# The last wait, the early routing and one weight piece moved in an xLSTM and mixture-of-experts kernel

## The chip, the core and the metric

The kernel runs on one core of a Trainium2 chip. A core has five engines with queues of their own: TensorE (PE), VectorE (DVE), ScalarE (ACT), GpSimd (POOL) and SyncE (SP, which only issues transfers here). The metric is the device time of one execution in microseconds (us), lower is better.

## What is computed

The input of the second stage is the output of the first.

```python
# stage 1, for B=2 batches, H=8 heads, S=768 steps, D=40
m_new = max(f + m, i);  C = exp(f+m-m_new)*C + exp(i-m_new)*outer(v, k);  n = the same with k
x = sigmoid(o) * (C @ q) / max(abs(n @ q), 1)          # x: [B, S, 320]
# stage 2, E=8 experts of width F=1024
logits = x @ w_gate;  local = sigmoid(x @ w_local)
e = argmax(logits) if s == 0 or local < 0.5 else the e of the step before
out[b, s] = softmax(logits)[e] * (relu(x @ w1[e]) @ w2[e])
```

## The kernel before

**Stage 1** goes through the sequence in six chunks (0 to 5) of 128 steps for all 16 pairs of batch and head. In a chunk TensorE makes exponents (`exponents(j)`, four quarters of four heads), ScalarE takes their exponentials, TensorE makes `scores`, VectorE multiplies both (`weigh(j)`), and TensorE makes the output of each quarter (`own_part(j)`, which reads the chunk's values) and what comes from the state (`old_part`). VectorE takes the outputs out of psO and adds both (`combine`, line 1459), keeps the state (`decay_state`, `add_state`) and makes x of the chunk before at the start of the next (`make_x`).

**Weights.** Every expert's weights come as five float32 pieces of 512 or 640 KB. ScalarE makes the float16 high half of a piece (`split_high`), VectorE the low half (`split_low`, line 1778), and only then is its staging slot free. `split_low` counts `weight_lows_ready` (s_wl) up by one. Pieces 0 to 19 are experts 0 to 3. The chunks do some of the low halves between their own steps: pieces 0 to 3 in chunk 1, 4 to 7 in chunk 2, 8 to 11 in chunk 3, 12 and 13 in chunk 4, 14 in chunk 5.

**Transfers.** SyncE issues its transfers in the order of the program, and a wait holds all that stand behind it. The loop of chunk c issues queries and keys of chunk c+1, the rows of x of chunk c-2, then a weight piece, then the values, keys and output gates of chunk c+1 (`in_kvo`, 968 KB), then the other pieces of `LOADS[c]`. A piece's load waits until the last user of its slot has its low half. So piece 8, the last load of chunk 1's loop, waits for the low half of piece 3 (s_wl 4); in chunk 2's loop piece 9 waits for that of piece 4, and the last, 12, for that of piece 7; piece 16, the last of chunk 3's loop, waits for that of piece 11 (s_wl 12), and piece 17, with the values of chunk 5 right behind it, for that of piece 12 (s_wl 13). Piece 18 waits for that of piece 15.

**GpSimd** scales the keys and splits the rows of exponents of the next chunk; `SPLIT_AT` is the count of low halves after which it starts the splitting. Later it gathers tiles of tokens from the x rows in HBM and writes tiles of the output, both by indirect transfers.

**Routing** of tokens to experts is made by VectorE with small products on TensorE. For chunks 0 to 2 it is done early, in chunks 4 and 5: `early_choice`, `early_fill` (needs the keys turned by TensorE), `early_codes` (needs TensorE's product of the codes), `early_slots` (needs that of the ranks), `early_sources`. The last writes `srcid`, with which GpSimd gathers the first tile. Then the same is done for all tokens (`route_choice`, `route_fill`, `route_codes`, `route_ranks`, `route_slots`).

**Stage 2** takes tiles of 128 tokens of one expert: `first_up` or `up` (up projection), relu, for the last tiles a `turn` (eight transposes) of the hidden row, then `down`, 24 products with float16 high and low halves of hidden and weights. The output tile is scaled and written by GpSimd.

```python
            turn(n3 + 2)                        # TensorE, the last tile
            idle(psM[:], GAP["last"])           # five products that nobody reads
            down(n3 + 2, e, halves=True)
            # GpSimd, after its last write
            pool.wait_ge(s_out, 16 * n3 + 48)
            pool.sem_inc(s_done, 1)
```

## Time and profile before

| | us |
|---|---|
| median of 3 runs (lowest, highest) | 232.96 (232.5, 234.62) |
| the profiled execution | 232.61 |
| its span, first to last instruction | 230.8 |
| TensorE matmul busy | 216.1 (94%) |
| VectorE busy | 168.1 (73%) |
| ScalarE busy | 122.8 (53%) |
| GpSimd busy | 68.2 (30%) |

The span is 1.8 us shorter than the time of the same execution. Stage 1 takes the first 97 us of the span, the routing of all tokens stands between 105 and 124 us under the first tiles, and the tiles run until 224 us. The mean granted clock of TensorE over the span is 0.996 of full speed.

### The profile page before, as it was taken

The numbers are of one execution on the slowest core, as the hardware profiler recorded it, in microseconds if no ns is written. First come the engines' busy times: TensorE is split into PE (matmuls) and PEld (weight loads), VectorE is DVE, ScalarE is ACT, GpSimd is POOL, SyncE is SP. The second block draws the span as 40 slices with busy tenths as digits, with TensorE's granted clock in tenths as the row PEclk, the third lists the DMA queues.
The fourth block names the chain that finished last, engine by engine and source line by source line (L and its number), as shares of the span: only waits on it lengthen the run. The fifth ranks groups of instructions, "written<-read, shape, count | busy, mean of one in ns | idle before, by whom it ended". The sixth has DMA issues, their size and how long they took to land.

```text
span 230.8 us, 5934 instructions
## 1 busy us (share of the span) xinstructions
PE 216.1 (94%) x2276; PEld 174.4 (76%) x2277; DVE 168.1 (73%) x348; ACT 122.8 (53%) x212; POOL 68.2 (30%) x77
## 2 busy tenths in 40 slices
PE   4998999999999899999999999999999999999970
PEld 1566878788888778899778698998889967666640
DVE  5599999999998989888898869998687630322130
ACT  2231769786968765455346727776666233334110
POOL 1043080260442430530013815431352332321021
PEclk9999999999999999999999999999999999999998
DMA  5999839999999720038940896896253011010000
GB/s 145 296 259 380 326 78 366 257 356 367 280 408 247 242 99 3 17 95 258 417 164 21 235 388 186 310 318 244 62 147 145 0 41 43 29 39 3 9 28 25
DMA packets 12840, 42.30 MB, mean 183 GB/s; under 512 B 2181, under 2 KB 4288, under 8 KB 12812
## 3 DMA queue, kind: packets, MB, share of 16 engines
q1 hardware_dynamic: 10812, 37.40, 48.4%
q0 software_dynamic: 1824, 4.35, 5.8%
q8 instruction: 19, 0.31, 0.6%
q10 hardware_dynamic: 176, 0.17, 0.3%
q14 instruction: 9, 0.07, 0.1%
HBM read 38.37 MB, written 4.98 MB: 188 GB/s over the span
## 4 chain that ended last, share of the span: by engine, by line
PE 73%; DVE 15%; DMA 4%; issue 3%; ACT 1%; POOL 0%; DVEq 0%; POOLq 0%
PE psU L1230 20%; PE psO L1049 7%; PE psO L1198 7%; PE psS L1198 6%; PE psS L1212 6%; PE psS L1019 4%; PE psU L1029 3%; PE psU L1101 2%; PE psU L899 2%; DVE W L1778 2%; PE psM L960 2%; PE psA L1000 2%; DMA stage<-in_w 2%; PE psA L1003 2%; PE psA L1005 2%
## 5 line engine op out<-in xcount | busy, mean ns | idle before, releaser
L1230 PE MATMUL psU<-W,hidT 128*128 128x320 f16 (+1 forms) x360 | 51.5, 299 | 0.1
L1230 PEld LDWEIGHTS psU<-W,hidT 128*128 128x128 f16 x360 | 35.0, 98 | 13.4 <-issue 0.5
L606 POOL DMA_INDIRECT out<-rows,srcid x11 | 15.1, 1375 | 56.3 <-ACT rows L828 56.0
L1049 PEld LDWEIGHTS psO<-W,hidT 128*128 128x128 f32 x192 | 24.1, 191 | 3.3 <-DVE hidT L1439 2.3
L1049 PE MATMUL psO<-W,hidT 128*128 128x82 f32 x192 | 25.6, 274 | 1.0 <-DVE W L1454 0.7
L1198 PE MATMUL psO<-xT,W 128*128 128x128 f16 x384 | 22.9, 219 | 0.0
L1198 PEld LDWEIGHTS psO<-xT,W 128*128 128x128 f16 x384 | 21.9, 98 | 0.4
L728 ACT ACTIVATE hid<-psA 128x512 f32<-128x512 f32 x24 | 14.2, 591 | 14.6 <-PE psA L1005 14.3
L1439 DVE TENSOR_TENSOR hidT<-psS,hid 128x512 f32<-128x512 f32 x24 | 16.4, 685 | 3.8 <-PE psS L1019 3.7
L558 POOL TENSOR_TENSOR W<-W 128x640 f32<-128x640 f32 x5 | 6.3, 1262 | 43.3 <-DVE W L1740 30.9
L1716 DVE TENSOR_TENSOR xT<-psM,xT 128x384 f16<-128x384 f32 x13 | 7.2, 557 | 14.7 <-ACT xT L720 14.6
L1198 PE MATMUL psS<-xT,W 128*128 128x128 f16 x256 | 15.1, 219 | 0.0
L1198 PEld LDWEIGHTS psS<-xT,W 128*128 128x128 f16 x256 | 14.6, 98 | 0.2
L1212 PE MATMUL psS<-W,xT 128*128 x64 | 14.5, 379 | 0.0
L1778 DVE SCALAR_TENSOR_TENSOR W<-W 128x1280 f16<-128x1280 f32 (+1 forms) x10 | 14.4, 1436 | 0.1
L1019 PE MATMUL psS<-W 40*128 40x128 f32 x192 | 13.9, 285 | 0.4 <-DVE hidT L1439 0.4
L1019 PEld LDWEIGHTS psS<-W 40*128 40x128 f32 x192 | 11.6, 187 | 3.2 <-issue 2.4
L828 ACT ACTIVATE rows<-psU,ptile 128x320 f32<-128x320 f32 x14 | 7.4, 527 | 10.9 <-PE psU L1230 8.1
L1778 DVE SCALAR_TENSOR_TENSOR W<-stage,W 128x1024 f16<-128x1024 f32 (+1 forms) x10 | 12.6, 1267 | 0.0
L662 ACT ACTIVATE W<-stage 128x1024 f16<-128x1024 f32 (+1 forms) x10 | 10.9, 1095 | 2.4 <-DMA stage<-in_w 2.4
L720 ACT CAST xT<-psM 128x384 f16<-128x384 f32 x13 | 6.2, 477 | 10.9 <-PE psM L1135 10.7
L662 ACT ACTIVATE W<-W 128x1280 f16<-128x1280 f32 (+1 forms) x10 | 11.8, 1180 | 0.1
(259 smaller groups left out, 436.3 us busy)
## 6 DMA issues: line engine op xcount, KB each, us to landing
W<-in_w SPq DMA_DIRECT2D x10, 512.0 KB, 5.5
W<-in_w SPq DMA_DIRECT2D x8, 640.0 KB, 6.5
W<-in_qk SPq DMA_DIRECT2D x12, 416.0 KB
W<-in_kvo SPq DMA_DIRECT2D x5, 968.0 KB, 7.6
stage<-in_w SPq DMA_DIRECT2D x9, 512.0 KB, 7.0
stage<-in_w SPq DMA_DIRECT2D x7, 640.0 KB, 7.3
rows<-in_w SPq DMA_DIRECT2D x5, 512.0 KB, 6.1
x_rows<-rows SPq DMA_DIRECT2D x12, 192.0 KB, 7.8
```

Of the source, the lines that this page charges most:

```text
L606: pool.indirect_dma_start(out[:, :], bass.IndirectOffsetOnAxis(ap=rows_of, axis=0), ybuf, None, bounds_check=TOK - 1, oob_is_err=False).th ...
L662: nc.scalar.activation(high(e, i), staged(n), ACT.Copy, scale=WSC).then_inc(s_wh, 1)
L728: nc.scalar.activation(wexp[j % 2], psA[:, j % 2], ACT.Exp).then_inc(s_exp, 1)
L828: nc.scalar.activation(ybuf, psU[:, 0:DM], ACT.Copy, scale=ptile[:, bass.ds(t, 1)]).then_inc(s_yk, 1)
L1019: last = mm(psS[:, a, h * P:(h + 1) * P], kstack[u][r, g], qstack[u][r, g], start=True, stop=True)
L1049: last = mm(psO[:, j % 2, h * V:(h + wide) * V], prob[j % 2][:, h], values, start=True, stop=True)
L1198: last = mm(at, W1[:, home(t), part, f * P:(f + 1) * P], x[:, k * P:(k + 1) * P], start=(n == 0), stop=(n == len(terms(t)) - 1))
L1212: last = mm(psS[:, half], x[:, k * P:(k + 1) * P], w, start=(n == 0), stop=(n == len(terms(t)) - 1))
L1230: return mm(psU[:, 0:DM], h[:, k * P:(k + 1) * P], w, start=(h is hi and part == 0 and k == 0), stop=(h is lo and k == FC - 1))
L1439: vv.tensor_tensor(prob[j % 2].rearrange("p h t -> p (h t)"), psS[:, j % 2], wexp[j % 2], ALU.mult).then_inc(s_p, 1)
L1716: vv.tensor_tensor(l, ps[:, 0:KC * P], h, ALU.subtract).then_inc(s_xte, 1)
L1778: vv.scalar_tensor_tensor(out=low(e, i), in0=staged(n)[p], scalar=WSC, in1=high(e, i)[p], op0=ALU.mult, op1=ALU.subtract).then_inc(s_wl, 1)
```

## The change

Five edits.

1. At the end VectorE, not GpSimd, waits for the last output writes.
2. The low half of piece 3 moves from chunk 1 to chunk 2, and with it one piece on every later boundary: chunk 1 does 0 to 2, chunk 2 does 3 to 6, chunk 3 does 7 to 10, chunk 4 does 11 and 12, chunk 5 does 13 and 14. `SPLIT_AT` goes down by one with it.
3. In chunk 4 TensorE makes the early codes after the state update and not ahead of `own_part(2)`, and the early ranks after the first scores of chunk 5 and not ahead of `own_part(3)`; each has a semaphore of its own. VectorE does `early_fill` after `combine(0)`, and `early_norms` at the end of chunk 5.
4. In the routing of all tokens VectorE does `route_fill` ahead of the first hidden low half and `route_codes` ahead of the early gates, and TensorE makes the slots one group of eight products later.
5. The last turn signals its first half, ScalarE starts on that, and the five idle products are gone.

```diff
-SPLIT_AT = (0, 0, A_CHUNK + 2, 2 * A_CHUNK + 2, 3 * A_CHUNK + 1)
+SPLIT_AT = (0, 0, A_CHUNK + 1, 2 * A_CHUNK + 1, 3 * A_CHUNK)
...
             for t in range(3):
                 write(n3 + t)
-            pool.wait_ge(s_out, 16 * n3 + 48)
-            pool.sem_inc(s_done, 1)
...
             def last_hidden_high(t):
-                act.wait_ge(s_ht, t + 1)
                 act.wait_ge(s_yh, t)
                 act.wait_ge(s_hk, t)
                 for half in range(2):
+                    act.wait_ge(s_ht, t + 1 + half)
...
-                mm(at_last1, r1["onesr"], r1["lastd"], start=True, stop=True)
+                mm(at_last1, r1["onesr"], r1["lastd"], start=True, stop=True).then_inc(s_cd1, 1)
...
                 pe.wait_ge(s_rv1, R1_OHB)
+                pe.wait_ge(s_oc, NQ * (NC - 1))
...
-                    if c == NC - 2 and j == 2:
-                        early_codes()
-                    if c == NC - 2 and j == 3:
-                        early_ranks()
...
                 scores(0)
+                if c == NC - 1:
+                    early_ranks()
...
                     last.then_inc(s_u, 1)
+                if c == NC - 2:
+                    early_codes()
...
-            def turn(t):
+            def turn(t, halves=False):
...
+                    if halves and k == FC // 2 - 1:
+                        last.then_inc(s_ht, 1)
...
-            first_up(3, {4: slots})
+            first_up(3, {5: slots})
...
-            turn(n3 + 2)
+            turn(n3 + 2, halves=True)
             e = expert(n3 + 2)
-            idle(psM[:], GAP["last"])
             down(n3 + 2, e, halves=True)
...
-                piece = A_CHUNK * (c - 1)
+                piece = A_CHUNK * (c - 1) - 1
...
                     combine(1)
-                    split_low(3)
                     return
...
                     weigh(2)
-                    early_fill()
                     combine(0)
                     scale_old(1)
                     keep_logits(2 * (c - 1))
+                    early_fill()
+                    weigh(3)
                     split_low(piece + 1)
-                    weigh(3)
                     early_codes()
...
-                    early_norms()
+                    split_low(piece - 2)
                     early_sources()
...
-                    split_low(piece - 2)
+                    split_low(piece - 1)
                     combine(1)
+                    early_norms()
...
+            route_fill()
             first_hidden_low(0)
-            route_fill()
             tile_low(2)
+            route_codes()
             early_gates()
-            route_codes()
             early_slot_gates()
             make_scale(NC - 1)
+            keep_gates(ptile[:, 0:LAST_E], at_gates1, s_gp1)
+            first_hidden_low(1)
             split_low(17)
-            first_hidden_low(1)
-            keep_gates(ptile[:, 0:LAST_E], at_gates1, s_gp1)
...
             result(n3 + 2)
+            dve.wait_ge(s_out, 16 * n3 + 48)
+            dve.sem_inc(s_done, 1)
```

VectorE from the end of chunk 1 to its first low half of chunk 2 (W is the memory of weights and attention, hidT holds the weighted scores, lg the logits). Before:

```order
L1459 TENSOR_TENSOR W<-psO,W 128x328 [waits old_part_scaled,outputs_ready]
L1778 SCALAR_TENSOR_TENSOR W<-W 128x4x320 [waits weight_highs_ready]
L1722 SCALAR_TENSOR_TENSOR W<-W 128x16 [waits outputs_taken]
L1725 TENSOR_SCALAR W<-W 128x16 [waits norm_bound_ready]
L1727 RECIPROCAL W<-W 128x16 [waits norm_bound_ready]
L1733 TENSOR_TENSOR W<-W 128x16x40 [waits norm_ready]
L1439 TENSOR_TENSOR hidT<-psS,hid 128x512 [waits outputs_ready,exp_done,scores_ready]
L1740 SCALAR_TENSOR_TENSOR W<-th,W 128x640 [waits x_transposed,x_rows_kept,output_gate_ready,normed_ready]
L1429 COPY lg<-psM 128x9 [waits logits_product_ready]
L1439 TENSOR_TENSOR hidT<-psS,hid 128x512 [waits outputs_ready,exp_done,scores_ready]
L1447 TENSOR_TENSOR W<-psU,W 128x328 [waits outputs_taken,old_part_ready]
L1778 SCALAR_TENSOR_TENSOR W<-W 128x4x320 [waits weight_highs_ready]
```

In the changed kernel:

```order
L1460 TENSOR_TENSOR W<-psO,W 128x328 [waits old_part_scaled,outputs_ready]
L1723 SCALAR_TENSOR_TENSOR W<-W 128x16 [waits outputs_taken]
L1726 TENSOR_SCALAR W<-W 128x16 [waits norm_bound_ready]
L1728 RECIPROCAL W<-W 128x16 [waits norm_bound_ready]
L1734 TENSOR_TENSOR W<-W 128x16x40 [waits norm_ready]
L1440 TENSOR_TENSOR hidT<-psS,hid 128x512 [waits outputs_ready,exp_done,scores_ready]
L1741 SCALAR_TENSOR_TENSOR W<-th,W 128x640 [waits x_transposed,x_rows_kept,output_gate_ready,normed_ready]
L1430 COPY lg<-psM 128x9 [waits logits_product_ready]
L1440 TENSOR_TENSOR hidT<-psS,hid 128x512 [waits outputs_ready,exp_done,scores_ready]
L1448 TENSOR_TENSOR W<-psU,W 128x328 [waits outputs_taken,old_part_ready]
L1779 SCALAR_TENSOR_TENSOR W<-W 128x4x320 [waits weight_highs_ready]
```

The instruction of line 1778 behind the last `combine` (the low half of piece 3) is gone there, and the one at the end of the second list, after `weigh(1)` and `scale_old(0)`, is now that of piece 3; SyncE's queue has no row moved.

TensorE in chunk 4 from the logits on (psO<-cfs,rows and psO<-W,rows are the codes, psU<-W 64x41 the state update). Before:

```order
L960 MATMUL psM<-W,xT 128x81 [waits x_transposed_kept,exp_done]
L960 MATMUL psM<-W,xT 128x81 x2
L973 MATMUL psO<-cfs,rows 128x6 [waits early_route_step,outputs_taken,weighted_scores_ready]
L974 MATMUL psO<-W,rows 128x6
L1049 MATMUL psO<-W,hidT 128x82 x4
L948 MATMUL psM<-cfs,W 128x128 [waits logits_kept,logits_product_ready,consts_loaded,decay_ready]
L948 MATMUL psM<-cfs,W 128x128
L948 MATMUL psM<-cfs,W 64x128
L1101 MATMUL psU<-W 64x41 [waits old_part_scaled,scaled_keys_ready]
L1101 MATMUL psU<-W 64x41 x15
L1000 MATMUL psA<-cbf,W 128x512 [waits exp_done,split_rows_ready]
```

In the changed kernel:

```order
L959 MATMUL psM<-W,xT 128x81 [waits x_transposed_kept,exp_done]
L959 MATMUL psM<-W,xT 128x81 x2
L1045 MATMUL psO<-W,hidT 128x82 [waits outputs_taken,weighted_scores_ready]
L1045 MATMUL psO<-W,hidT 128x82 x3
L947 MATMUL psM<-cfs,W 128x128 [waits logits_kept,logits_product_ready,consts_loaded,decay_ready]
L947 MATMUL psM<-cfs,W 128x128
L947 MATMUL psM<-cfs,W 64x128
L1099 MATMUL psU<-W 64x41 [waits old_part_scaled,scaled_keys_ready]
L1099 MATMUL psU<-W 64x41 x15
L972 MATMUL psO<-cfs,rows 128x6 [waits early_route_step]
L973 MATMUL psO<-W,rows 128x6
L1000 MATMUL psA<-cbf,W 128x512 [waits exp_done,split_rows_ready]
```

The two codes products now stand behind the state update, and `own_part(2)` follows the logits directly.

VectorE in chunk 4 from the low half ahead of `weigh(2)` to the first step of the codes. Before:

```order
L1778 SCALAR_TENSOR_TENSOR W<-W 64x1024 [waits weight_highs_ready]
L1439 TENSOR_TENSOR hidT<-psS,hid 128x512 [waits outputs_ready,exp_done,scores_ready]
L1611 TENSOR_SCALAR rows<-psO 6x128 [waits outputs_ready]
L1612 SCALAR_TENSOR_TENSOR rows<-rows,psO 6x128 [waits early_route_step]
L1613 TENSOR_SCALAR W<-cfs,rows 6x6 [waits early_route_step]
L1459 TENSOR_TENSOR W<-psO,W 128x328 [waits old_part_scaled,outputs_ready,x_ready,early_route_step]
L1447 TENSOR_TENSOR W<-psU,W 128x328 [waits outputs_taken,old_part_ready]
L1429 COPY lg<-psM 128x9 [waits logits_product_ready]
L1778 SCALAR_TENSOR_TENSOR W<-W 128x4x320 [waits weight_highs_ready]
L1439 TENSOR_TENSOR hidT<-psS,hid 128x512 [waits outputs_ready,exp_done,scores_ready]
L1618 TENSOR_SCALAR W<-psO 128x6 [waits outputs_ready]
```

In the changed kernel:

```order
L1779 SCALAR_TENSOR_TENSOR W<-stage,W 128x1024 [waits weight_highs_ready]
L1440 TENSOR_TENSOR hidT<-psS,hid 128x512 [waits outputs_ready,exp_done,scores_ready]
L1460 TENSOR_TENSOR W<-psO,W 128x328 [waits old_part_scaled,x_ready,outputs_ready]
L1448 TENSOR_TENSOR W<-psU,W 128x328 [waits outputs_taken,old_part_ready]
L1430 COPY lg<-psM 128x9 [waits logits_product_ready]
L1612 TENSOR_SCALAR rows<-psO 6x128 [waits outputs_ready]
L1613 SCALAR_TENSOR_TENSOR rows<-rows,psO 6x128 [waits early_route_step]
L1614 TENSOR_SCALAR W<-cfs,rows 6x6 [waits early_route_step]
L1440 TENSOR_TENSOR hidT<-psS,hid 128x512 [waits exp_done,outputs_ready,scores_ready,early_route_step]
L1779 SCALAR_TENSOR_TENSOR W<-W 64x1024 [waits weight_highs_ready]
L1619 TENSOR_SCALAR W<-psO 128x6 [waits early_codes_turned]
```

`combine(0)` (W<-psO,W) now stands three steps earlier, and the second low half, whose end is s_wl 13, stands behind `early_fill` and `weigh(3)`.

## Rows read from the trace of the kernel before

**Rows 1.** The page: the chain of waits by engine, share of the span.

```profile
PE 73%; DVE 15%; DMA 4%; issue 3%; ACT 1%; POOL 0%; DVEq 0%; POOLq 0%
```

**Rows 2.** Timeline, VectorE, chunk 2: start us, us, instruction.

```profile
41.82 0.68 DVE L1439 TENSOR_TENSOR hidT<-psS,hid 128x512 f32<-128x512 f32 x1
...
44.23 1.78 DVE L1778 SCALAR_TENSOR_TENSOR W<-W 128x1280 f16<-128x1280 f32 x1
```

**Rows 3.** Timeline, TensorE, the start of chunks 2 and 3.

```profile
39.68 1.16 PE L1019 MATMUL psS<-W 40*128 40x128 f32 x16
...
42.56 1.12 PE L1049 MATMUL psO<-W,hidT 128*128 128x82 f32 x8 [0.23 <-DVE hidT L1439]
...
57.05 1.09 PE L1049 MATMUL psO<-W,hidT 128*128 128x82 f32 x8
```

**Rows 4.** Timeline, SyncE's queue, chunks 1, 2 and 4.

```profile
40.48 0.33 SPq L473 DMA_DIRECT2D W<-in_w  x1
...
46.42 0.58 SPq L463 DMA_DIRECT2D W<-in_kvo  x1
...
76.81 0.33 SPq L473 DMA_DIRECT2D W<-in_w  x1
...
77.18 0.43 SPq L463 DMA_DIRECT2D W<-in_kvo  x1
```

**Rows 5.** DMA issues from 40.3 on (piece 8): KB, us to landing.

```profile
W<-in_w SPq DMA_DIRECT2D x1, 640.0 KB, 5.5
```

**Rows 6.** DMA issues at 103.7 (piece 18).

```profile
stage<-in_w SPq DMA_DIRECT2D x1, 640.0 KB, 4.6
```

**Rows 7.** DMA issues at 46.4 (values of chunk 3).

```profile
W<-in_kvo SPq DMA_DIRECT2D x1, 968.0 KB, 8.5
```

**Rows 8.** DMA issues at 77.1 (values of chunk 5).

```profile
W<-in_kvo SPq DMA_DIRECT2D x1, 968.0 KB, 5.9
```

**Rows 9.** Busy time from 41 to 54: us, PE busy, clock, DMA share, GB/s.

```profile
41.00:54.00 13.00, 12.77 (x135) 1.00 0.95 322
```

**Rows 10.** Timeline, TensorE, chunk 4 and the start of chunk 5.

```profile
79.24 0.19 PE L973 MATMUL psO<-cfs,rows 6*128 6x6 f32 x1 [0.88 <-DVE W L1459]
...
87.58 0.38 PE L903 MATMUL psA<-cbf 128*128 128x512 bf16 x1
```

**Rows 11.** Timeline, VectorE, chunk 4.

```profile
77.42 0.27 DVE L1611 TENSOR_SCALAR rows<-psO 6x128 f32<-6x128 f32 x1
...
78.64 0.50 DVE L1459 TENSOR_TENSOR W<-psO,W 128x328 f32<-128x328 f32 x1
...
79.73 1.48 DVE L1778 SCALAR_TENSOR_TENSOR W<-W 128x1280 f16<-128x1280 f32 x1
```

**Rows 12.** Timeline, VectorE, the low half of the first tile.

```profile
98.65 0.56 DVE L1716 TENSOR_TENSOR rows<-psA,rows 128x384 f16<-128x384 f32 x1 [0.70 <-ACT rows L720]
```

**Rows 13.** Timeline, TensorE: first gathered tile, keys, slots.

```profile
97.55 0.55 PE L1135 MATMUL psA<-cfs,xt 128*128 128x128 f32 x3 [0.21 <-DMA xt<-x_rows,srcid]
...
108.17 0.27 PE L1152 MATMUL psA<-cfs,W 128*12 128x128 f32 x1
...
123.77 0.46 PE L1168 MATMUL psA<-W 128*128 128x16 bf16 x12 [0.52 <-DVE W L1898]
```

**Rows 14.** Timeline, VectorE, the first low half of a hidden tile.

```profile
107.96 1.22 DVE L1800 SCALAR_TENSOR_TENSOR hidT<-psS,hidT 128x1024 f16<-128x1024 f32 x1
```

**Rows 15.** Timeline, the last tile: ScalarE and GpSimd.

```profile
219.29 1.07 ACT L820 CAST hidT<-psO 128x512 f16<-128x512 f32 x2 [3.11 <-PE psO L1220]
...
225.25 0.98 POOL L606 DMA_INDIRECT out<-rows,outid  x1 [2.38 <-DVE rows L1818]
```

**Rows 16.** Chain of waits, the last tile: start us, us, what.

```profile
218.38 0.87 PE psO L1220 x8
...
219.26 1.08 PE psM L908 x5
```

**Rows 17.** The instructions after the last line of the program, GpSimd.

```profile
L98 POOLq DRAIN  x1: 2770/2770/2770, 227.8 to 227.8; - x1
```

More of the change, by code:

```diff
@@ L67 @@
 LOADS = {1: (5, 6, 7, 8), 2: (9, 10, 11, 12), 3: (13, 14, 15, 16), 4: (17, 18)}
-GAP = dict(tile=1, last=5)
+GAP = dict(tile=1)
 BIG = 2.0 ** 30
@@ L72 @@
 G_L0, G_B0, G_L1, G_A1, G_B1, G_L, G_A, G_B, G_EG = 5, 12, 16, 18, 19, 23, 25, 26, 27
-R1_KEY, R1_SUB, R1_KEPT, R1_OHB, R1_HOT, R1_SRC, R1_END = 8, 9, 12, 17, 28, 34, 44
+R1_KEY, R1_SUB, R1_KEPT, R1_OHB, R1_HOT, R1_SRC, R1_END = 8, 9, 12, 17, 28, 30, 44
 R_KEY, R_SUB, R_CODE, R_OHB, R_HOT, R_SRC, R_REST, ROUTE_STEPS = 10, 11, 14, 19, 46, 48, 67, 73
@@ L303, in build @@
         s_yh = sem("high_products_done")
+        s_cd1, s_rk1 = sem("early_codes_turned"), sem("early_ranks_ready")
         s_cb, s_tab = sem("bf16_consts_loaded"), sem("router_weights_loaded")
@@ L973, in early_codes @@
                 nc.tensor.transpose(at_code1, r1["coder"], const("ident")[0:N1, 0:N1])
-                mm(at_last1, r1["onesr"], r1["lastd"], start=True, stop=True)
+                mm(at_last1, r1["onesr"], r1["lastd"], start=True, stop=True).then_inc(s_cd1, 1)
             def early_ranks():
                 pe.wait_ge(s_rv1, R1_OHB)
+                pe.wait_ge(s_oc, NQ * (NC - 1))
                 mm(at_later1, trib, r1["ohb"][:, 0:LAST_E * N1], start=True, stop=True)
-                mm(at_total1, sel_ones, r1["ohb"][:, 0:LAST_E * N1], start=True, stop=True)
+                mm(at_total1, sel_ones, r1["ohb"][:, 0:LAST_E * N1], start=True, stop=True).then_inc(s_rk1, 1)
             def early_slots():
@@ L1660, in early_codes @@
             def early_codes():
-                dve.wait_ge(s_o, NQ * (NC - 2) + 3)
+                dve.wait_ge(s_cd1, 1)
                 carry(early, r1, N1, at_code1, at_last1)
@@ L1666, in early_slots @@
             def early_slots():
-                dve.wait_ge(s_o, NQ * (NC - 1))
+                dve.wait_ge(s_rk1, 1)
                 hot_of = r1["ohb"][:, 0:LAST_E * N1]
```

## The prediction

> **What bounds the kernel now.** I read the chain of waits first, then the timelines of TensorE and VectorE side by side over stage 1, then SyncE's queue, then the last tile. The chain is TensorE for 73% of the span, VectorE 15%, transfers 4% [rows 1]: work that TensorE does itself can't be touched by this change, so what it can win is the idle time between. The reader is to see four such places. At the start of chunk 2 TensorE waits 0.23 for the first weighted scores [rows 3]. In chunk 4 it waits 0.88 for `combine(0)` [rows 10]. At the slots it waits 0.52 [rows 13]. In the last tile five products that nobody reads take 1.08 [rows 16]. After the program GpSimd drains for 2.77 [rows 17]. No transfer stops TensorE in stage 1 except the first gather, 0.21 [rows 13], but SyncE's queue was hardly ever empty: from 41 to 54 the DMA engines were 95% busy at 322 GB/s [rows 9].
>
> **The change part by part.** A minus is time saved; positions are those of the profiled execution.
>
> Chunk 1. The low half of piece 3 stood on VectorE ahead of `make_x` and `weigh(0)` of chunk 2, which started at 41.82 [rows 2]; a low half of that form takes 1.48 [rows 11]. Without it `weigh(0)` starts when the scores are there: they start at 39.68 and take 1.16 [rows 3], so at 40.9. TensorE then has its filling products, and `own_part(0)` starts at 42.15, not 42.56: the 0.23 of idle and the rest that the model of the matmul ends hides. Term: **-0.4**.
>
> SyncE's queue, the price of the move. The low half also frees a slot. SyncE issued piece 8 at 40.48 [rows 4], when that of piece 3 ended. Now this low half stands where that of piece 4 stood, at 44.23 [rows 2], less the 0.9 that VectorE is ahead: it runs from 43.3 and ends, with 1.5 to 1.8 for it, at 45.0. Queries and keys of chunk 3, the rows, piece 9 and the values of chunk 3 are queued behind piece 8, and all move by 4.5 at first. Before, the values were issued at 46.42 and landed 8.5 later, at 54.9 [rows 4, 7], 14.4 after the issue of piece 8; of these 0.9 were an older backlog (piece 8 took 5.5 to land, a like piece in an empty queue 4.6 [rows 5, 6]). So upper bound: 45.0 + 13.5 = 58.5. Lower bound: these transfers are 3.55 MB (640, 832, 384, 640 and 968 KB), at 322 GB/s [rows 9] 11.0, and 1 for the start: 57.0. I take 58.0, nearer to the upper, which is the same list in the same order. `own_part(0)` of chunk 3 needs the values, at 57.05 before [rows 3], at 56.65 now. Term: **+1.3** (0.4 to 1.9), a new wait of TensorE on a transfer; it stands at +0.9 then.
>
> Chunk 4 has the same queue (piece 12 now waits for a low half of chunk 3), but its values come at 71 to 72.5 by the same sum from 59.5, and TensorE, 0.9 late, asks for them at about 72.4: nothing.
>
> Chunk 4, codes and ranks. `early_fill` took from 77.42 to 78.64 and `combine(0)` came after it [rows 11]; TensorE waited 0.88 for it until 79.24 and made the codes before `own_part(2)` [rows 10]. Now `combine(0)` is first, `own_part(2)` can start when the logits end, 1.3 earlier, and the two groups of small products come back later at 0.2: **-1.1**. VectorE gives back half of this, since it does the same list, but one low half is 1.22 and not 1.48; it is not late at the next chunk.
>
> Chunk 5, the same queue again. Piece 17 went at 76.81 and the values at 77.18, landing 5.9 later, at 83.1 [rows 4, 8]; TensorE asked for them at 87.58 [rows 10], so 4.5 were to spare. Now s_wl 13 is the second low half of chunk 4. From 77.42: `combine(0)`, `scale_old`, logits 1.1 (78.64 to 79.73 [rows 11]), `early_fill` 1.2, `weigh(3)` 0.6, low half 1.25, end 81.6. Values go at 82.05, land at the earliest at 87.95 (5.9 [rows 8]), plus the 0.9 by which all is late: 88.9. Upper bound: piece 16 now goes at 76.8, where piece 17 went, and with queries, keys, rows, piece 17 and values it is 3.29 MB, by the same rate as in chunk 3 (13.5 for 3.55) 12.5: 89.3, and 90.2 with the 0.9. I take 89.5, the middle. TensorE is then 1.9 later than at 87.58 before; without the wait it would be at 0.9 - 1.1 = 0.2 earlier. Term: **+2.1** (1.5 to 2.8). The spare time is spent because the wait moved past a whole block of `early_fill`, `weigh` and a low half.
>
> The Trainium skill bears on this: "DMA: Bandwidth & Descriptors", section on the anatomy of one DMA, gives for a GpSimd transfer about 2.0 us fixed plus bytes over 436 GB/s. By that estimate the 968 KB land 4.3 after issue, or 5.5 with the 512 KB ahead of them, and the wait of chunk 5 nearly vanishes; the row shows 5.9.
>
> End of chunk 5. `early_sources` gets a low half of 1.48 before it and loses `early_norms` (0.85) and a wait of 0.2; the gather that follows ended a wait of 0.21 [rows 13]: +0.15. `early_norms` now stands between `combine(1)` and the first tile's low half, where VectorE waited 0.70 for ScalarE [rows 12]: 0.85 is 0.2 too much. Together **+0.35** (0 to 0.6).
>
> All tokens' routing. Eight products later are 0.45 against the wait of 0.52 [rows 13]. But VectorE now waits for the keys before the first hidden low half: it started that at 107.96 [rows 14], the keys only ran at 108.17 for 0.27 [rows 13], so 0.5 is idle where before 0.2 was (for tile 2's high half). The slots come 0.3 later. Term: **-0.25** (-0.5 to 0).
>
> Last tile. Before, ScalarE began at 219.29 after the whole turn, two copies in 1.07 [rows 15], and the five products took 1.08 from 219.26 [rows 16]. The turn took 0.87 for eight transposes [rows 16]; now the first four are enough: ScalarE starts at 218.85, its half is there at 219.4, and `down` starts at 219.45, not 220.33. VectorE's half is needed 16 products later. Term: **-0.85**.
>
> The end. The last indirect transfer runs at 225.25 for 0.98 [rows 15], GpSimd sees it landed and only then drains, 2.77 from 227.8 [rows 17]. Now it can drain from 226.25 while the data are on the way, and VectorE sees them when GpSimd did. Not shown is a drain with a transfer in flight: if it waits for that, 0 is gained; if not, 1.55. GpSimd had nothing to run for 1.5 before its drain and it still took 2.77, so it isn't left-over work: I take **-1.55**.
>
> Sum: -0.4 + 1.3 - 1.1 + 2.1 + 0.35 - 0.25 - 0.85 - 1.55 = -0.4. The profiled execution's 232.61 gives 232.2; the median of the runs is 0.35 above it, so 232.5. About 1% is what a measurement of this kernel can tell from no change.
>
> **Rivals.**
> (a) The transfers are hidden. For it: 4.5 were to spare in chunk 5, and an emptied queue may be quicker than a full one. Against it: the 5.9 was already in a nearly empty queue. Then there are no +1.3 and little of +2.1, TensorE is 1.5 ahead at chunk 5, VectorE's path to the gather only 0.9: -0.9 - 0.25 - 0.85 - 1.55 = -3.5, 229.5. The page's rule above leads here.
> (b) Slower: the queue of SyncE costs its upper bounds. Chunk 3's values at 58.5 make TensorE 1.45 late, chunk 5's then come at 90.75, 3.2 late: 3.2 + 0.35 - 0.25 - 0.85 - 1.55 = +0.9, 233.9. It decides from a landing of chunk 5's values after 89.9. For it: queries and keys come in the middle of the list each time.
> (c) GpSimd's drain waits for the transfer: 1.55 not gained, 234.0.
> (d) The new order doesn't remove the wait of chunk 4, since VectorE is the bound there: +1 on the forecast, but most of that would only shorten the wait on chunk 5's values. It hardly changes the sum.
>
> **How the numbers follow.** Forecast 0.53 (232.5, from 231 to 233.5 by the terms' bounds), (a) 0.18, (b) 0.14, (c) 0.15. The range from 229.7 to 234.2 leaves out about half of (a) and the worst of (b) and (c). Faster by over 1% (below 230.6) is (a) and a little of the forecast, 0.22; slower by over 1% (above 235.3) is (b) and (c) together, 0.1; the rest, 0.68, within 1%.
>
> **What the profile after would show.** SyncE's queue: piece 8 at 45, the values of chunk 5 at about 83. TensorE: waits for `in_kvo` at the first own part of chunk 3 (about 1.3) and chunk 5 (about 2), none for `combine(0)` in chunk 4, still one at the slots of some 0.5, and none of the five products. GpSimd's drain starting near the end of its last transfer. I am wrong above all if these two waits on the values aren't there, or if the drain ends where it did.

## The result: slower, 244.2 us

| | before | changed |
|---|---|---|
| median of 6 runs each (lowest, highest), us | 232.8 (232.5, 234.62) | 244.17 (240.16, 245.3) |
| ratio, 95% interval | | 1.0385 [1.03, 1.047] |
| the profiled execution | 232.61 | 244.6 |
| its span | 230.8 | 242.8 |
| mean granted clock of TensorE | 0.996 | 0.954 |

The ratio is made only from runs within 1.5% of the fastest of each kernel (240.16, 242.18 and 243.74 us of the changed one), so it lies below that of the two medians, and the profiled 244.6 us is one of the three left out. The forecast was 232.5 us, within 229.7 to 234.2: it was wrong by 11.7 us.

I read the profile after in the order of before. First the chain of waits by engine, for [rows 1]:

```profile
PE 70%; DVE 13%; DMA 11%; issue 3%; SPq 1%; POOLq 1%; ACT 0%; DVEq 0%; ACTq 0%
```

Transfers went from 4% of the chain to 11%. The chain in order of time names them, two loads of `in_kvo` (start us, us, what):

```profile
50.27 11.97 DMA W<-in_kvo
...
89.29 9.14 DMA W<-in_kvo
```

Next SyncE's queue, for [rows 4]. A group of issues of one line is one row: start of the first, us until the end of the last.

```profile
38.92 8.81 SPq L474 DMA_DIRECT2D W<-in_w  x2
47.82 0.36 SPq L455 DMA_DIRECT2D W<-in_qk  x1
...
50.27 0.47 SPq L464 DMA_DIRECT2D W<-in_kvo  x1
...
74.86 9.43 SPq L474 DMA_DIRECT2D stage<-in_w  x2
84.39 0.35 SPq L455 DMA_DIRECT2D W<-in_qk  x1
...
89.29 0.48 SPq L464 DMA_DIRECT2D W<-in_kvo  x1
```

Piece 8 is the second of the two issues from 38.92 on and ends at 47.73. Between them SyncE stands still for 8 us, with the queries and keys of chunk 3 and its values behind it. In chunk 3's loop the same happens to piece 16 (until 84.29), with chunk 5's queries, keys and values behind it. TensorE pays for both, for [rows 3, 10, 13]:

```profile
41.96 1.16 PE L1019 MATMUL psS<-W 40*128 40x128 f32 x16
...
62.29 2.00 PE L1045 MATMUL psO<-W,hidT 128*128 128x82 f32 x8 [3.43 <-DMA W<-in_kvo]
...
92.97 1.21 PE L1019 MATMUL psS<-W 40*128 40x128 f32 x16 [1.31 <-DMA W<-in_qk]
...
98.48 0.61 PE L902 MATMUL psA<-cbf 128*128 128x512 bf16 x1 [2.32 <-DMA W<-in_kvo]
...
111.32 0.55 PE L1135 MATMUL psA<-cfs,xt 128*128 128x128 f32 x3 [0.37 <-DMA xt<-x_rows,srcid]
...
138.10 0.46 PE L1168 MATMUL psA<-W 128*128 128x16 bf16 x12 [0.89 <-DVE W L1899]
...
233.54 3.52 PE L1232 MATMUL psU<-W,hidT 128*128 x24 [0.40 <-ACT hidT L819]
```

The three waits on transfers are 7.1 us. That is not all that was lost: the eight products of `own_part` that took 1.09 in [rows 3] take 2.00 here. The windows show why (us, then busy us of PE, PEld, DVE, ACT and POOL with counts, granted clock, DMA share, GB/s):

```profile
35.94:39.35 3.41, 3.41 (x42) 2.88 (x40) 3.28 (x7) 3.41 (x8) 0.00 (x0) 0.50 0.99 398
59.83:66.66 6.83, 4.37 (x21) 3.52 (x23) 3.65 (x7) 3.41 (x8) 4.02 (x5) 0.50 0.93 296
93.97:104.20 10.23, 7.91 (x46) 6.65 (x44) 4.45 (x16) 2.87 (x8) 0.41 (x1) 0.50 0.21 83
```

These are three stretches in which TensorE's granted clock is 0.50, that is 1.2 GHz and not 2.4. Two of them hold a wait on a transfer or follow one: the first fell after TensorE had waited some 1 us of its 3.43, the second 1 us after the wait on the keys. TensorE was busy for 15.7 us in the three; at full clock that would be about half, so by this estimate some 7.8 us are lost by the clock: 1.7 in the first stretch, which stands ahead of any wait on a transfer, and 6.1 in the other two. Before, the clock was at 0.50 only from 228.9 us on, after the last product.

The lag behind the profiled execution of before, at the same instruction in both, puts it together (my differences of the two traces' start times):

| place | before | changed | lag |
|---|---|---|---|
| transposes of x, chunk 1 | 34.77 | 35.54 | 0.77 |
| first scores of the next chunk | 39.68 | 41.96 | 2.28 |
| `own_part(0)`, chunk 3 | 57.05 | 62.29 | 5.24 |
| `own_part(0)`, chunk 4 | 71.53 | 78.81 | 7.28 |
| `own_part(3)`, chunk 4 | 82.92 | 89.06 | 6.14 |
| products ahead of `own_part(0)`, chunk 5 | 87.58 | 98.48 | 10.90 |
| first gathered tile | 97.55 | 111.32 | 13.77 |
| last `down` | 220.17 | 233.54 | 13.37 |
| end of the span | 230.8 | 242.8 | 12.0 |

The first 2.28 us are not the moved piece's doing: 0.77 stand there from the first products of the program on (5.86 us for 14 of them, 5.07 before), and 1.5 come with the first stretch at half clock; both belong to the section on the clock in chunk 1. The 1.1 that chunk 4 was to give is there (7.28 to 6.14), and 1.4 at the end too (13.37 to 12.0); from the first gathered tile to the last `down` it gains 0.4. Everything else loses.

The end, for [rows 15, 17] (GpSimd's last transfer, then the instructions after the program's last line):

```profile
238.71 0.98 POOL L607 DMA_INDIRECT out<-rows,outid  x1 [1.96 <-DVE rows L1819]
...
L98 POOLq DRAIN  x1: 4055/4055/4055, 238.5 to 238.5; - x1
L98 DVEq DRAIN  x1: 17/17/17, 241.3 to 241.3; - x1
```

From the start of the last transfer to the end of the span it is 4.1 us, where it was 5.55 (225.25 to 230.8).

### The profile page after: what moved, and what is told of

It is laid out like the page before. It is cut to its first block, busy times and chain, and to the rows that moved or that the text cites. A ratio compares the mean times of both kernels' runs of the same rounds, so it can differ in the third digit from the quotient of the medians.

```text
span 242.8 us, 5925 instructions
## 1 busy us (share of the span) xinstructions
PE 222.9 (92%) x2271; PEld 180.1 (74%) x2272; DVE 167.9 (69%) x348; ACT 123.5 (51%) x212; POOL 68.2 (28%) x77
## 3 DMA queue, kind: packets, MB, share of 16 engines
HBM read 38.37 MB, written 4.98 MB: 179 GB/s over the span
## 4 chain that ended last, share of the span: by engine, by line
PE 70%; DVE 13%; DMA 11%; issue 3%; SPq 1%; POOLq 1%; ACT 0%; DVEq 0%; ACTq 0%
PE psU L1232 19%; DMA W<-in_kvo 9%; PE psO L1198 8%; PE psS L1198 7%; PE psO L1045 6%; PE psS L1212 6%; PE psS L1019 4%; PE psU L898 2%; DVE W L1779 2%; PE psM L959 2%; PE psU L1029 2%; PE psA L1000 2%; PE psU L1099 2%; PE psA L1003 2%; PE psA L1005 2%
## 5 line engine op out<-in xcount | busy, mean ns | idle before, releaser
L1232 PEld LDWEIGHTS psU<-W,hidT 128*128 128x128 f16 x360 | 35.1, 98 | 13.5 <-issue 0.6
L1045 PE MATMUL psO<-W,hidT 128*128 128x82 f32 x192 | 27.2, 286 | 4.2 <-DMA W<-in_kvo 3.4
L1045 PEld LDWEIGHTS psO<-W,hidT 128*128 128x128 f32 x192 | 26.1, 204 | 6.4 <-DMA W<-in_kvo 3.6
L559 POOL TENSOR_TENSOR W<-W 128x640 f32<-128x640 f32 x5 | 7.4, 1481 | 53.8 <-DVE W L1741 31.2
L1019 PE MATMUL psS<-W 40*128 40x128 f32 x192 | 15.0, 299 | 1.8 <-DMA W<-in_qk 1.3
L1019 PEld LDWEIGHTS psS<-W 40*128 40x128 f32 x192 | 12.6, 201 | 5.0 <-issue 2.5
L591 POOL DMA_INDIRECT xt<-x_rows,srcid x6 | 7.9, 1323 | 14.7 <-DVE srcid L1694 12.4
L1029 PE MATMUL psU<-W 104*128 104x82 f32 x80 | 12.0, 297 | 0.0
```

What stands on the lines that cost most here:

```text
L591: pool.indirect_dma_start(xbufs[x_buffer(t)], None, xs[0:count], bass.IndirectOffsetOnAxis(ap=rows_of, axis=0), bounds_check=count - 1, oo ...
L1019: last = mm(psS[:, a, h * P:(h + 1) * P], kstack[u][r, g], qstack[u][r, g], start=True, stop=True)
L1029: last = mm(old.rearrange("p (a h) d -> p h a d", a=2)[:, i], qstack[u][0:PAIR, g], Cbd[0:PAIR, g], start=True, stop=True)
L1045: last = mm(psO[:, j % 2, h * V:(h + wide) * V], prob[j % 2][:, h], values, start=True, stop=True)
L1232: return mm(psU[:, 0:DM], h[:, k * P:(k + 1) * P], w, start=(h is hi and part == 0 and k == 0), stop=(h is lo and k == FC - 1))
```

## The experiments

The theories after the result: **the queue** (SyncE, held by the moved low halves, brings values and keys late, and TensorE's clock falls in the waits), against **VectorE's order** (codes, fill and norms in their new places make it late), against a clock that falls by itself. Each kernel was compared with runs of the kernel before on the same chip; its medians there were 234.85 us (beside the first four kernels), 234.74 (the next four) and 235.46 (the last three), higher than in the first comparison. What goes with that is told with the last runs.

### The weight piece put back, all else kept

```diff
-SPLIT_AT = (0, 0, A_CHUNK + 1, 2 * A_CHUNK + 1, 3 * A_CHUNK)
+SPLIT_AT = (0, 0, A_CHUNK + 2, 2 * A_CHUNK + 2, 3 * A_CHUNK + 1)
...
-                piece = A_CHUNK * (c - 1) - 1
+                piece = A_CHUNK * (c - 1)
...
                     combine(1)
+                    split_low(3)
...
-                    split_low(piece - 2)
                     early_sources()
...
-                    split_low(piece - 1)
+                    split_low(piece - 2)
```

> The changed kernel with the weight piece back where it was (low half of piece 3 in chunk 1, pieces of the later chunks as before); every other edit is kept. Theory 1, the queue: SyncE's list is held by the moved low halves, so chunk 3's and chunk 5's values (and chunk 5's keys) land late. Then TensorE's waits on transfers in chunks 3 and 5 (3.43, 1.31 and 2.32 us) and the stretches at half clock are gone, and what is left is the forecast's sum without -0.4, +1.3 and +2.1: +0.35 - 1.1 - 0.25 - 0.85 - 1.55 = -3.4, that is 229.4 us beside 232.8. Theory 2, VectorE: codes, ranks, fill and norms in the new order make VectorE late for TensorE in chunks 4 and 5, and the queue only follows it. Then some 240 us or more.

Measured: 232.24 us (229.34 to 232.34, 4 runs), ratio 0.9868 [0.9798, 0.9939]. TensorE's idle places from 33 to 110 us are two:

```profile
34.83 0.90 PE L947 MATMUL psM<-cfs,W 128*128 128x128 f32 x3 [0.63 <-DVE W L1424]
...
98.99 0.55 PE L1135 MATMUL psA<-cfs,xt 128*128 128x128 f32 x3 [0.28 <-DMA xt<-x_rows,srcid]
```

No wait on keys or values is left. The loss of the change is the moved piece; VectorE's order as the cause has fallen. The one run with a mean clock of 0.994 took 229.34, which is the forecast of 229.4; the other three had 0.982 to 0.983 and took 232.2 to 232.3. The profiled execution is one of the three: its clock was at 0.50 for 6.8 us in chunk 1. From `own_part(0)` of chunk 3 (59.61) to the end of its span (230.4) it is 170.8 us, before 173.8 (57.05 to 230.8): by positions the edits that are left gave 2.9 us and not 3.4, so that the 229.34 meets the forecast so closely is in part luck.

### The weight piece alone

The same lines the other way, on the kernel before.

> The kernel before with the weight piece moved and nothing else. Theory 1, the queue: the values of chunk 3 land some 12 us after their issue, late by 3 us or more, and chunk 5's also; the time is that of the changed kernel plus the 3.4 that the other edits give: some 247 us (244 to 249). Theory 2, VectorE's new order in chunks 4 and 5 is the cause: only chunk 3's wait is there, and the time is under 240 us.

Measured: 251.78 us (249.14 to 255.13, 4 runs), ratio 1.0622 [1.0543, 1.0701]. The waits, and then the window behind the first of them:

```profile
63.09 2.00 PE L1049 MATMUL psO<-W,hidT 128*128 128x82 f32 x8 [3.40 <-DMA W<-in_kvo]
...
100.97 1.16 PE L1019 MATMUL psS<-W 40*128 40x128 f32 x16 [0.76 <-DMA W<-in_qk]
...
106.38 0.61 PE L903 MATMUL psA<-cbf 128*128 128x512 bf16 x1 [3.20 <-DMA W<-in_kvo]
```

```profile
62.00:82.40 20.40, 19.31 (x117) 16.67 (x117) 8.22 (x14) 8.26 (x16) 4.88 (x6) 0.50 0.76 242
```

The waits are 7.4 us, against 7.1 in the changed kernel, so the moved piece makes them by itself. Two of the four runs took 249.1 and 249.3 us, at the upper end of my 244 to 249; the other two, the profiled one with 254.27 among them, lie above it. In that trace the clock was at 0.50 for 30.7 us in stage 1 and not for 20.5: 6.8 in chunk 1, 20.5 at the first wait (61.9 to 82.4), 3.4 at the end of the last one (106.3 to 109.7). The sum that I made from the changed kernel took the length of such a stretch for fixed, and it isn't.

### Values ahead of the pieces in SyncE's list

```diff
-LOADS = {1: (5, 6, 7, 8), 2: (9, 10, 11, 12), 3: (13, 14, 15, 16), 4: (17, 18)}
+LOADS = {1: (5, 6, 7), 2: (8, 9, 10, 11), 3: (12, 13, 14, 15), 4: (16, 17, 18)}
...
-                    load_piece(LOADS[c][0])
                     load_values(c + 1, (c + 1) % 2)
-                    for n in LOADS[c][1:]:
+                    for n in LOADS[c]:
```

> The changed kernel with SyncE's list turned round: each chunk's values ahead of its weight pieces, and the piece that had stood first in the list left for the next chunk (pieces 5-7, 8-11, 12-15, 16-18). VectorE's order is the changed one. Theory 1, the queue: the values are asked for early enough, TensorE doesn't wait for them in chunks 3 and 5, the clock stays at full, and the time is 229 to 231 us, if the last pieces are still there for the first tile. Theory 2, VectorE's order: the wait moves from the values to weighted scores or the state, and the time stays above 238 us.

Measured: 230.85 us (229.02 to 232.16, 4 runs), ratio 0.9834 [0.9758, 0.9909]. VectorE's order is the changed one, with the late low halves. SyncE now has the values of chunk 3 out at 42.2 and lets piece 8 wait behind them:

```profile
42.17 0.60 SPq L464 DMA_DIRECT2D W<-in_kvo  x1
47.60 2.19 SPq L474 DMA_DIRECT2D W<-in_w  x2
```

No wait on keys or values is in the trace, only one of 0.69 for the first gather (98.83). So it isn't the late low half that costs, but what stands behind it in the queue. From `own_part(0)` of chunk 5 to the first gather it is 10.25, and 9.82 in the kernel with the piece put back: the 0.4 are the low half that now stands ahead of `early_sources`.

### TensorE kept busy in the waits

```diff
+COVER = {3: 14, 5: 10}
...
+                    if c in COVER:
+                        fill(0, COVER[c])
                     pe.wait_ge(s_kvo[u], 16 * (k + 1))
```

> The changed kernel with products that nobody reads ahead of TensorE's wait for the values in chunk 3 (14 of them) and chunk 5 (10), so that TensorE is busy while it would wait. Theory A, the clock falls because TensorE stands still, and work after the wait pays for it: the two stretches at 0.50 (6.8 and 10.2 us) get shorter or vanish, and the time is 238 to 241 us. Theory B, the waits themselves are the whole price, or the clock falls for another reason: 244 us as before or more, with the stretches at 0.50 in their places.

Measured: 238.6 us (236.14 to 240.06, 4 runs), ratio 1.0134 [1.0057, 1.0212]. The profiled execution took 236.14; its clock was at 1.00 until the end:

```profile
59.83:66.66 6.83, 6.58 (x62) 5.81 (x62) 3.08 (x5) 5.06 (x10) 4.69 (x6) 1.00 0.89 246
93.97:104.20 10.23, 9.90 (x92) 8.54 (x89) 7.48 (x20) 4.37 (x12) 3.71 (x3) 1.00 0.07 18
```

TensorE in chunks 1 to 3 and at the start of chunk 5 (line 903 is the fill):

```profile
39.57 1.16 PE L1020 MATMUL psS<-W 40*128 40x128 f32 x16
...
42.05 1.01 PE L1046 MATMUL psO<-W,hidT 128*128 128x82 f32 x8
...
56.31 3.19 PE L903 MATMUL psA<-cbf 128*128 128x512 bf16 x14
60.08 1.12 PE L1046 MATMUL psO<-W,hidT 128*128 128x82 f32 x8 [0.58 <-DMA W<-in_kvo]
...
88.44 1.16 PE L1020 MATMUL psS<-W 40*128 40x128 f32 x16 [1.04 <-DMA W<-in_qk]
...
90.53 2.65 PE L903 MATMUL psA<-cbf 128*128 128x512 bf16 x11
93.01 1.01 PE L1046 MATMUL psO<-W,hidT 128*128 128x82 f32 x8
```

The same work runs 8.5 us shorter than the changed kernel's profiled execution (244.6) with 24 products more. Not all of that is the filling's: 0.9 us are the start of the program (14 products in 4.98 and 5.86 us), and some 1.7 the fall of the clock in chunk 1, which this execution didn't have. The medians are 5.6 us apart (238.6 and 244.17), near the 6.1 estimated for the two stretches after waits. The rest is the waits: 236.14 stands 6 to 7 us above the 229.0 and 229.8 of the profiled executions of the two mended kernels at the end of this section. So of the moved piece's loss about half is the clock and half the waits. This is also the trace that shows the waits without the clock in between: 3.7 us in chunk 3 (14 products of 0.22 and 0.58), 1.0 for the keys and some 2.2 for the values of chunk 5 (the values land at 92.7, and TensorE had nothing else to do from 90.5 on).

SyncE here issues piece 8 at 45.0 (a row of 38.04 with 7.30 for two issues) and the values at 47.97; they land 12.1 later, at 60.0.

### Four small edits, each alone on the kernel before

> The kernel before, with VectorE instead of GpSimd waiting for the last writes. Theory 1: GpSimd's drain runs beside its last transfer; from the issue of the last indirect transfer to the end of the program it takes 4.0 us, as in the changed kernel, where it was 5.55: -1.5 us. Theory 2: the drain gets longer by what it no longer waits beforehand, or VectorE's sight of the landing is later: 0. TensorE's last group ends at the same place in both.

Measured: 233.28 us (230.84 to 234.03, 12 runs), ratio 0.9922 [0.9872, 0.9971].

```profile
227.26 0.98 POOL L606 DMA_INDIRECT out<-rows,outid  x1 [2.36 <-DVE rows L1816]
...
L98 POOLq DRAIN  x1: 4081/4081/4081, 227.0 to 227.0; - x1
```

From 227.26 to the span's end of 231.3 it is 4.0, before 5.55: -1.5. The drain got longer, from 2.77 to 4.08, but not by what it no longer waits beforehand.

> The kernel before, with the last turn released in two halves and the five products that nobody reads taken out. Theory 1: TensorE's last products start 0.85 us earlier after the end of the first up products of that tile (ScalarE's copy of the first half no longer waits for the last four transposes): -0.8 us. Theory 2: without the five products TensorE stands still for some 0.5 us and the last products run at half clock for longer than before (3.9 us at the end of the kernel before): 0, or slower by up to 1.

Measured: 233.74 us (231.95 to 235.54, 12 runs), ratio 0.9968 [0.9919, 1.0018].

```profile
220.36 1.04 PE L1220 MATMUL psO<-cfs,hid 128*128 128x128 f32 x8
221.80 3.57 PE L1232 MATMUL psU<-W,hidT 128*128 x24 [0.40 <-ACT hidT L820]
```

From the turn's first transpose to `down` it is 1.44, before 1.95 (218.22 to 220.17): -0.5. ScalarE's copy began 0.72 after the turn's start and `down` 0.72 after that. The last products didn't run at half clock, and neither did they before: the 3.9 us of the expectation begin at 228.9, after the last product.

> The kernel before, with the early codes and ranks later on TensorE and the early fill behind the weighted sum on VectorE, without the moved weight piece. Theory 1: TensorE's wait of 0.88 us for the weighted sum in chunk 4 is gone and the first gather comes earlier by some 1 us: -0.8 to -1.1 us. Theory 2: VectorE's list is as long as it was and sets when the first gather's indices are ready, so that TensorE's wait moves to the gather (0.21 us before): -0.2 us at most.

Measured: 233.77 us (231.87 to 234.69, 12 runs), ratio 0.9962 [0.9919, 1.0004].

```profile
74.13 1.09 PE L1047 MATMUL psO<-W,hidT 128*128 128x82 f32 x8
...
89.22 1.01 PE L1047 MATMUL psO<-W,hidT 128*128 128x82 f32 x8
...
99.13 0.55 PE L1137 MATMUL psA<-cfs,xt 128*128 128x128 f32 x3 [0.37 <-DMA xt<-x_rows,srcid]
```

From `own_part(0)` of chunk 4 to that of chunk 5 it is 15.09, before 16.28 (71.53 to 87.81): -1.2, and 0.2 of it are given back at the gather (9.91 against 9.74).

> The kernel before with only the new order on VectorE after stage 1 (the keys' fill ahead of the first hidden low half, the codes ahead of the early gates) and the slots' products eight products later on TensorE. One look, for positions: from the first gathered tile's transposes (97.55 before) to the slots' products (123.77) it was 26.2 us, to the second tile's products (129.96) 32.4. Forecast's theory: the wait at the slots stays at some 0.5 and the way to 129.96 gets shorter by 0.25. Rival: VectorE waits for the keys for longer than it gains, the slots' wait grows to 0.9, as in the changed kernel's variants, and the way is not shorter (32.4 to 32.6).

Measured: 235.74 us, one run.

```profile
100.37 0.55 PE L1135 MATMUL psA<-cfs,xt 128*128 128x128 f32 x3 [0.31 <-DMA xt<-x_rows,srcid]
...
127.06 0.46 PE L1168 MATMUL psA<-W 128*128 128x16 bf16 x12 [0.88 <-DVE W L1898]
...
132.80 2.47 PE L1230 MATMUL psU<-W 128*128 128x320 f16 x17 [0.25 <-issue]
```

The way from the first gathered tile to the second one's products is 32.43, before 32.41. The slots' products stand eight products later and are still waited for, 0.88 instead of 0.52: the rival held. VectorE stood idle for 0.62 before the keys that it now takes first:

```profile
111.37 0.28 DVE L1611 TENSOR_SCALAR W<-psA 12x128 f32<-12x128 f32 x1 [0.62 <-PE psA L1152]
```

Of the three edits with twelve runs only the end's has an interval clear of 1; the sizes of the other two are from the traces.

### The clock in chunk 1

Runs of one kernel differed by 3 us. In eight of the ten profiles shown so far (all but that of the kernel before and that with the waits filled) the clock fell at 35 us of the span, at 34.6 to 36.5, for 3.4 or 6.8 us. A wait of 0.62 for VectorE stands there in every one, in the kernel before too. Three products, 0.65 us, were put in front of it, on each of three kernels:

```diff
+EARLY_COVER = 3
...
+                if c == 1:
+                    fill(2, EARLY_COVER)
                 if c > 0:
                     x_transposes(2 * (c - 1) + 1, 1, c - 1)
```

On the kernel with values first:

> The changed kernel with the values ahead of the pieces in SyncE's list, and three products that nobody reads on TensorE in chunk 1, ahead of the transposes for which it waits 0.63 us at 35 us of the span. In three of the four profiled variants with a changed list the clock fell to half right there, for 3.4 or 6.8 us. Theory A, the fall follows the idle time: with it filled the clock stays at full until the end in nearly all runs, and the median goes from 230.9 to 229.0 us (the two runs of that kernel with a mean clock of 0.994 or more took 229.0 and 229.6). Theory B, the fall has nothing to do with this idle time: the runs keep falling into the two groups of 229 and 232 us.

(At the time of the expectation it was four of five variants: with the piece alone it fell too.) Measured: 229.91 us (229.02 to 230.49, 6 runs), ratio 0.9783 [0.9726, 0.984]. All six runs have a mean clock of 0.993 or more, as theory A says, but only three took 229.0 to 229.4; the other three took 230.4 to 230.5.

On the kernel with the piece back:

> The changed kernel with the weight piece back, and the three filling products ahead of the 0.63 us wait in chunk 1. If the clock's fall at 35 us of the span follows that idle time, all runs have a mean clock of 0.993 or more, and the time is that of the undisturbed run of the kernel without the products, 229.3 us, not 232.2. Theory V: turning SyncE's list round (values first) is worth something of its own beyond undoing the move; then this kernel is slower than the 229.0 to 229.4 of the values-first kernel by 0.5 us or more. Theory W: with the queue never late, the list doesn't matter, and both are within 0.3 us.

Measured: 229.56 us (229.19 to 230.06, 4 runs), ratio 0.9796 [0.971, 0.9882]. All four runs have a mean clock of 0.993 or more. The medians with the two lists are 0.35 us apart, near theory W's 0.3, and this kernel is not the slower one: theory V has fallen.

On the kernel before:

> The kernel before with the three filling products in chunk 1 alone. Its runs beside the experiments fell into groups by mean clock: 232.5 to 233.1 us at 0.995, 234.5 to 235.0 at 0.988, 235.5 to 236.2 at 0.976. If the groups are the fall of the clock in chunk 1 (none, 3.4 us long, 6.8 us long), all runs are now at 232.3 to 233.1 us. If not, the groups stay.

Measured: 233.85 us (233.13 to 234.25, 10 runs) beside a median of 235.46 of the kernel before; ratio 0.9958 [0.9922, 0.9993]. The window in chunk 1 of the kernel with the piece back, without and then (second fence) of the kernel before with the three products:

```profile
35.00:38.00 3.00, 3.00 (x37) 2.26 (x38) 2.90 (x6) 3.00 (x7) 0.00 (x0) 0.50 0.91 359
```

```profile
35.00:38.00 3.00, 3.00 (x48) 2.24 (x46) 2.83 (x8) 3.00 (x8) 0.00 (x0) 1.00 0.87 283
```

In all three profiles there is no fall in chunk 1, and no run of the three kernels was 2 us or more above its fastest. The groups of the kernel before are gone as well, and with them one that the expectation left out: of its 49 runs beside the experiments 11 took 232.5 to 233.1 us, 17 took 234.0 to 235.0, 17 took 235.5 to 236.2, and four took 243.0 to 245.1 with a mean clock of 0.940 to 0.946. No trace of those four was kept, so why the kernel before at times is as slow as the changed one stays open. But on the kernel before I had forecast 232.3 to 233.1 and the median was 233.85. The profiled execution shows 0.75 of that at its very start, in the 14 products that start the program. Here first the kernel before, then the same with the three products:

```profile
3.21 5.07 PE L899 MATMUL psU<-cbf 128*128 128x512 bf16 x14 [3.21 <-DMA cbf<-in_cb]
```

```profile
3.17 5.82 PE L900 MATMUL psU<-cbf 128*128 128x512 bf16 x14 [3.17 <-DMA cbf<-in_cb]
```

The same products took 4.49 in the profile of the values-first kernel with the three products. They are the same in every kernel, so this is run to run and no effect of an edit; whether it explains the median of all ten runs I can't show, since only one of them has a trace.

That start goes with what happens in chunk 1. Side by side, the traces of all kernels fall into bands:

| profiles | first 14 products, us | clock at 0.50 in chunk 1 |
|---|---|---|
| kernel before, waits filled | 5.07, 4.98 | none |
| piece back, piece alone, codes alone, routing alone | 5.22 to 5.28 | 6.8 us |
| changed, values first, end alone, halves alone | 5.86 to 6.16 | 3.4 us |
| the three with products ahead of the wait | 4.49, 5.26, 5.82 | none |

The bands hold for kernels with quite different edits, so whether the clock falls in chunk 1, and for how long, went with the start of the execution and not with an edit; that is a pattern of ten traces, no experiment. The three products are an experiment: 5.26 lies in the band of the 6.8 us falls and 5.82 at the edge of the other, and neither trace has one. The third, 4.49, lies outside both bands and proves less. For the main comparison it means that the profile of before was one without the fall and that of the changed kernel one with it.

## Why the prediction was wrong

**The mechanism was forecast, the sign of the sum was not.** SyncE's queue being held, the new waits on `in_kvo` in chunks 3 and 5, piece 8 issued at 45.0 (it was 45.01 where no clock fell), chunk 4's values without a wait, the end of the wait for `combine(0)`: all are in the trace. Rival (b), which named this mechanism with a price of 233.9, was right in kind and short by 10 us. Three steps failed.

1. **A missing term: the clock.** The prediction turned a wait of TensorE into a loss of the same length. Waits on transfers of 3.4 us, and of 1.3 and 2.3 us together, took the clock to 0.50 for 6.8 and 10.2 us, and in the kernel with the piece alone one of 3.4 took it there for 20.5. That cost about 6.1 us of the changed kernel's profiled execution, and the fall in chunk 1 another 1.7; filling the waits made the median 5.6 us shorter. [rows 9] show a clock of 1.00, so the profile of before had no price for it: after the start of the program TensorE's longest idle time there was 0.88 [rows 10], and the forecast brought in waits of 1.3 and 2.1. The Trainium skill, "TensorE: Matmul & The Clock Gate", section on HAM oscillation, describes a kernel whose products start at half rate after each wait on a transfer, and prices that at half of the throttled time. The trace agrees if only the busy time is counted: 15.7 of the 20.5 us at half clock, so 7.8, against the 8.5 between the two profiled executions less the 0.9 of their starts, 7.6.

2. **"Term: +1.3 (0.4 to 1.9)" for chunk 3** was 3.7 at full clock and 3.43 in the changed kernel. The values were to land at 58.0, at most 58.5; they landed at 60.0, 15.0 after piece 8's issue and not 13.0 to 13.5. The upper bound took 0.9 off the 14.4 of before, for a queue that starts empty; nothing came off. The lower bound counted 3.55 MB ahead of the values. What moved between piece 8's issue and the landing was 298 GB/s for 15.0 us, 4.5 MB, and before it was 326 for 14.4, 4.7 MB: by these bytes the pieces queued behind the values share the engines with them and belong in the sum; no run took them away to show it. The list took its 14 to 15 us in all three traces (14.4, 15.0 and, in the changed kernel, 14.9), wherever it started. (For chunk 4 the same sum, from 59.5, gives 71.5 to 73.0 and not the 71 to 72.5 of the prediction; no trace has a wait there.)

3. **"Term: +2.1 (1.5 to 2.8)" for chunk 5** was 1.0 for the keys and 2.2 for the values at full clock. The values' issue was right once chunk 3's true wait is carried on (82.05 forecast and 3.0 late there, 85.03 measured); the landing took 7.7 and not 6.6. The wait on the keys was not in the prediction: `in_qk` stands behind piece 16 like the values, and I followed only the values.

The profiled execution was forecast at 232.2 and took 244.6, 12.4 us more. The wait terms, 6.9 for 3.4, are 3.5 of that, the clock after the waits 6.1, the clock in chunk 1 1.7 and the start of the program 0.8; the small terms below missed by 0.7 together. That makes 12.8, within 0.4 of the 12.4. The fall in chunk 1 and the start, 2.5 us together, come from no edit.

**The small terms** held in sign, mostly in size. Chunk 1, -0.4: at full clock the scores and `own_part(0)` stand 2.48 apart, before 2.88 [rows 3]. Codes and ranks, -1.1: -1.2. End of chunk 5, +0.35: +0.5 with the moved low half where nothing else is late (values first), +0.1 with the waits filled, +0.2 or less without it. Routing, -0.25: 0, the wait at the slots grew to 0.9 as VectorE idled 0.6 for the keys. Last tile, -0.85: -0.5; I let `down` start 0.6 after ScalarE's copy began and that 0.63 after the turn's first transpose, both take 0.72, and the start that I took for before, 220.33, was 220.17 in the timeline. The end, -1.55: -1.5, rival (c) has fallen. But the number is right in part by luck: I had GpSimd's drain start 1.0 after its last transfer and last 2.77; it started 0.2 ahead of that row and took 4.06 to 4.08. Without the piece's terms the sum was to be -3.4. By times it came out at -3.5 (229.34 against the 232.8 of the first comparison), by positions at -2.9, and the parts measured above, -1.2, +0.2, 0, -0.5 and -1.5, make -3.0.

Rival (a), transfers hidden, was the furthest from what happened. The estimate of 4.3 to 5.5 us for the values, worked out in the prediction from the page "DMA: Bandwidth & Descriptors" of the Trainium skill, section on the anatomy of one DMA, stands against 12.0 and 9.1 in the changed kernel and 12.1 and 7.7 in the one with the waits filled; the page gives it per transfer on GpSimd's path, and here it was one of a list on SyncE's.

## What to carry to other kernels

Before a wait moves, write down everything that stands behind it in its queue and how long the whole list takes to land with what follows it; if the first thing that TensorE asks for stands behind a transfer that waits for a buffer, put it in front: that, with one piece left for the next loop, turned +3.9% into -1.7%, with the same late buffers. Where TensorE is busy nearly all the time, a new idle stretch can cost nearly twice its length (here 6.9 us of waits and some 6.1 of clock), and a few products that nobody reads are a cheap test of whether that is so. Of a change with several edits, the ones on the fixed path (the drain, the order of small products) can be summed from the trace within 0.4 us each; a wait on a shared queue can't, and its upper bound should be no less than the whole list as it ran before (14.4 us here, and it took 15.0), with nothing taken off. And before two profiles are compared, compare their first products: the start alone differed by up to 1.7 us, and a fall of the clock went with it.

## What the runs showed of the hardware

- The stretch at half clock at a wait was 6.8, 10.2, 20.5 or 3.4 us long, for waits of 3.4, 1.3 with 2.3, 3.4 and 3.2 us. In the longest TensorE was busy for 19.3 of 20.4 us at 1.2 GHz, and it still lasted.
- The clock also fell in chunk 1, where TensorE stood still for 0.62 us only. The runs of the kernel before fall into groups at 232.5 to 233.1 (mean clock 0.995), 234.0 to 235.0 (0.983 to 0.988), 235.5 to 236.2 (0.975 to 0.977) and, four of 49, 243.0 to 245.1 us (0.940 to 0.946). In ten traces the fall went with the time of the first 14 products: none at 4.98 and 5.07 us, 6.8 us long at 5.22 to 5.28, 3.4 us long at 5.86 to 6.16. With three products of 0.22 us ahead of the idle time there was none at 5.26 and 5.82 either.
- The 14 products that start the program took 4.49 to 6.16 us in different profiles. In a kernel of 230 us that is 0.7%.
- GpSimd's drain took 4.06 and 4.08 us beside a transfer in flight, and 2.77 after waiting until it had landed. It began beside the transfer, and was 1.3 us longer for it.
